# Twenty-two dummy products on TensorE ahead of the first expert tile

## The reference

```python
def _moe_ref(x, w_gate, w_local, w1, w2):
    ...
            h = np.maximum(x[b, s] @ w1[e], 0.0)
            out[b, s] = p[e] * (h @ w2[e])

def _moe2_ref(x, g_ln, w_ch1, w_ch2):
    ...
    xn = (x - mu) / np.sqrt(var + 1e-06) * g_ln
    ch = np.maximum(xn @ w_ch1, 0.0) @ w_ch2
    return (x + ch).astype(np.float32)
```

## Time and profile before

| | |
|---|---|
| median of three runs | 433.4 us |
| span of the profiled execution, first to last instruction | 428.4 us |
| rest of the time, by that median | 5.0 us |
| TensorE products, busy | 392.5 us (92%) |
| VectorE, ScalarE, GpSimd busy | 233.5, 139.4, 127.5 us |
| mean granted TensorE clock | 0.944 |

### The profile page before, as it was taken

The page is one execution under the profiler, slowest core; times in us unless marked ns, Lnnn a source line. Parts: engine busy times, 40 slices in busy tenths (PEclk is TensorE's granted clock), DMA queues, the critical chain, the costliest instruction groups (busy, mean ns, idle before and its releaser), DMA issues.

```text
span 428.4 us, 7294 instructions
## 1 busy us (share of the span) xinstructions
PE 392.5 (92%) x2640; PEld 372.0 (87%) x2640; DVE 233.5 (54%) x440; ACT 139.4 (33%) x283; POOL 127.5 (30%) x128
## 2 busy tenths in 40 slices
PE   6799999995049999999999999899999999999993
PEld 5799999894049999999999999788998899988993
DVE  6887879974406573663745769586303652133110
ACT  0424536320007254372553735452002220022000
POOL 4685653613705235053250521300100001100010
PEclk9999999955559999999999999999999999999998
DMA  7998984063534869577584270410010001000000
GB/s 114 154 248 209 249 213 73 20 227 124 203 116 148 256 228 364 178 271 261 201 314 159 102 261 1 128 59 2 18 38 18 0 2 37 27 13 2 18 20 37
DMA packets 62250, 54.77 MB, mean 128 GB/s; under 512 B 41216, under 2 KB 56960, under 8 KB 62208
## 3 DMA queue, kind: packets, MB, share of 16 engines
q1 hardware_dynamic: 47744, 19.58, 18.8%
q10 hardware_dynamic: 12032, 26.74, 18.1%
q0 software_dynamic: 2432, 7.92, 4.8%
HBM read 43.13 MB, written 11.10 MB: 127 GB/s over the span
## 4 chain that ended last, share of the span: by engine, by line
PE 82%; DVE 6%; issue 4%; DMA 3%; ACT 2%; SPq 1%; POOL 0%; DVEq 0%; ACTq 0%; POOLq 0%
PE bank L1200 21%; PE bank L1202 21%; PE bank L1201 21%; PE bank L1162 4%; PE bank L1159 3%; PE bank L1147 3%; PE bank L1137 2%; PE bank L1171 2%; PE bank L1113 2%; PE bank L1195 1%; DMA kn<-in_k 1%; PE bank L1126 1%; DVE split L365 1%; PE bank L1212 1%; DMA xrow<-xsort 1%
## 5 line engine op out<-in xcount | busy, mean ns | idle before, releaser
L360 ACT CAST split<-raw 128x1024 fp32r<-128x1024 f32 (+1 forms) x60 | 59.2, 1004 | 0.0
L1200 PE MATMUL bank<-xT,split 128*128 128x256 f32 x192 | 55.1, 287 | 2.1 <-DVE xT L901 2.1
L1202 PE MATMUL bank<-xT,split 128*128 128x256 f32 x192 | 54.8, 286 | 0.0
L1201 PE MATMUL bank<-xT,split 128*128 128x256 f32 x192 | 54.8, 286 | 0.0
L365 DVE TENSOR_TENSOR split<-raw,split 128x1024 fp32r<-128x1024 f32 (+1 forms) x40 | 52.9, 1337 | 1.8 <-ACT split L360 1.7
L590 POOL DMA_INDIRECT out<-orow,cpos x12 | 11.6, 970 | 133.4 <-DVE orow L1030 133.4
L1200 PE MATMUL bank<-split,h2T 128*128 128x384 f32 x144 | 48.7, 338 | 0.0
L1202 PE MATMUL bank<-split,h2T 128*128 128x384 f32 x144 | 48.2, 335 | 0.0
L1201 PE MATMUL bank<-split,h2T 128*128 128x384 f32 x144 | 48.1, 334 | 0.0
L365 POOL TENSOR_TENSOR split<-raw,split 128x1024 fp32r<-128x1024 f32 (+1 forms) x20 | 45.8, 2305 | 5.7 <-ACT split L360 3.4
L1042 DVE SCALAR_TENSOR_TENSOR h2T<-bank,h2T 128x512 fp32r<-128x512 f32 x36 | 24.9, 691 | 38.0 <-ACT h2T L702 37.8
(11 more groups left out here) (166 smaller groups left out, 764.3 us busy)
## 6 DMA issues: line engine op xcount, KB each, us to landing
raw<-in_w ACTq DMA_DIRECT2D x14, 1536.0 KB, 7.3
raw<-in_w_ch ACTq DMA_DIRECT2D x2, 2304.0 KB, 9.0
xsort<-zeros SPq DMA_DIRECT2D x8, 388.0 KB
X<-xsort SPq DMA_DIRECT2D x8, 388.0 KB, 5.8
ysort<-yrow POOLq DMA_DIRECT2D x8, 388.0 KB, 7.0
raw<-in_w SPq DMA_DIRECT2D x2, 1536.0 KB, 8.2
X<-ysort SPq DMA_DIRECT2D x3, 776.0 KB, 6.2
rn<-in_r SPq DMA_DIRECT2D x12, 192.0 KB, 4.8
```

Source lines behind the costliest of these rows:

```text
L360: act.copy(hi, src).then_inc(s_hi, 1)
L1200: pe.matmul(dst, stationary[0], moving[0], start=first, stop=False)
L1201: pe.matmul(dst, stationary[0], moving[1], start=False, stop=False)
L1202: return pe.matmul(dst, stationary[1], moving[0], start=False, stop=last)
```

## The change

A loop of 22 bf16 products is put on TensorE between `expert_regs` and the first tile's transposes. Each has `blank` (128x128 zeros) as its stationary operand and the same tile, repeated four times, as its 512 moving columns, and writes bank 0. Nobody reads what they write: the transposes overwrite it. They carry no wait and no signal.

```diff
     WARM_UP = 56
+    KEEP_WARM = 22
...
             pe.sem_inc(m_o, WT)
             tiles, before, _, behind, more = expert_regs(pe)
 
+            for _ in range(KEEP_WARM):
+                pe.matmul(bank[0][:], blank[:], blank[:].unsqueeze(1).broadcast_to([P, 4, P]), start=True, stop=True)
+
             def moe_transpose():
```

## The result

Ten executions of each gave a median of 435.86 us for the changed kernel and 433.5 us for the one before. The ratio of the two is 1.0067, with a 95% interval from 1.0048 to 1.0086: slower by 2.9 us, and clear of no change. One of the changed kernel's ten took 678.23 us at a mean granted clock of 0.548, and the ratio is of the other nine. Timed again in a later series, the changed kernel came to 436.43 us, ratio 1.0090 [1.0058, 1.0122].

What follows compares the result with a forecast made beforehand. TensorE was taken to set the end, busy 295.4 of 296.6 us from 125.22. Transposes 5.8 us later less 2.0 given back make +3.8, 428.4 to 432.2; with 5.0 around the span, 437.2 us, range 435.8 to 439.3.

Steps and rivals of the forecast that it cites:

- the forecast's own +3.0 to +5.0: The main case's range of loss in us at the end of the profiled execution, given 72 in 100.
- Where the dummies start: TensorE's hole before the first transposes: dummies start near 120.5 behind the tenth read; only 1.1 us to 121.59 is free.
- What they take: The 22 dummies: 9.6 products in 4.07 us, 12.4 in 2.80, 6.87 us in all; transposes 5.8 us later.
- What is given back: First transposes and expert products at full clock: 0.72 us plus 1.28 us, together 2.0 us.
- The rule of the Trainium skill: First six transposes: full clock does not engage, so the 0.72 us would be missing and the sum +4.5 us.
- The products' 1.28 us: First expert products: 13.7 take 1.64 us at full clock in place of 2.92, 1.28 us less.
- The clock that falls again: Rival, between dummies and first products: clock falls, +5.1, at worst +6.4 us, 438.5 to 439.8 us; 12 in 100.
- Absorbed downstream: Rival: TensorE's one later wait, on VectorE's normalised rows, absorbs up to 1.2 us, giving 436.0 us; 6 in 100.
- The sum: End of the profiled execution: 5.8 - 2.0 = +3.8 us, 428.4 to 432.2, giving 437.2 us.
- the 5.0 us between span and median: Time taken to lie around the profiled span by the median, added to the span to forecast the measured time.
- Faster, same: Rivals: dummies start at 113.3, hidden, 431.4 us, 3 in 100; start between 115.7 and 117.7, no change, 3 in 100.
- the estimate from the Trainium skill: The ten reads: about 200 ns per register load, ending at 115.3, dummies near 122.2; -1.4 us, 432.0 us.

Runs made afterwards that it cites:

- the run with narrow dummies: 22 dummies of 128 columns in place of 512, at the changed kernel's place behind the reads; 431.73 against 432.49 us, ratio 0.9981.
- The run with the start at 115.0: The changed kernel's 22 dummies behind the second of the ten reads in place of the tenth; 432.28 against 432.49 us, ratio 0.9993.

## Why the prediction was right, point by point

The mechanism was right: the dummies start behind the tenth read, run past the rows and are paid for on TensorE. Of the number, part is luck. The measured 435.86 us is 2.5 us above the 433.4 that the forecast started from; it lies 0.06 us above the lower end of the range, and below the forecast's own +3.0 to +5.0. That lower end is lower than its working gives: +3.2 less the half microsecond is +2.7, or 436.1 us, and the text has 435.8. The forecast of 437.2 us itself is 1.3 us too high.

**Where the dummies start.** Forecast: right behind the tenth read, near 120.5, with 1.1 us free. Measured: 120.5 in the later series, 122.5 in the first profile, whose attention ended 1.58 us later. Right, and the run with the 22 behind the second read shows that this start decides.

**What they take.** Forecast 6.87 us, with the rise after 4.07. Measured 6.76 and, in the later series, 7.41 us (the rise after 3.7 and 5.1), and 12.18 for 44 where the same rates give 6.87 + 22 x 0.226 = 11.8. The transposes came 5.95 and 6.55 us later against the last routing product; the forecast was 5.8.

**What is given back.** Forecast 2.0 us. Measured 2.0 where the clock stayed, 0.5 where it fell (299.91 less 297.92 and 299.41). Transposes 0.82 for 1.54 us, as forecast. The rule of the Trainium skill ("TensorE: Matmul & The Clock Gate", Part 4: PE-mode transpose) that the full clock does not engage for them is not borne out in any of the runs that reached them at 1.00. The products' 1.28 us: from the first product to the last of all, 295.0 us with the clock at 1.00 throughout against 296.28 before, 1.26 less.

**The clock that falls again.** A rival with 12 in 100, and the chance that I mis-sized. Four profiles reached the transposes at 1.00 with the pause behind them empty (the changed kernel twice, the one with 44 behind the reads, the 22 behind the second read), and the clock fell in three: in the pause in the last, 0.4 to 1.1 us behind the first product in the other two. I had argued from the earlier trace rows, a stretch with a pause of 1.7 us in which the clock stayed at 1.00. That was one execution. In five of the experiments' profiles the clock fell in this same stretch, between 11.0 and 11.6 us, and in the changed kernel's first at 13.6. The run with 22 ahead of the reads, for one:

```profile
7.70:12.10 4.40, 1.80 (x12) 0.94 1.26 193
```

The price was over-estimated in turn: a fall takes back 1.5 us (296.51 against 295.02), hardly more than the products' 1.3, and not up to twice that. With that pause filled the clock fell in neither of two profiles.

**Absorbed downstream.** This rival's 436.0 us is the number nearest to the measured one, but it is not what happened. The wait that was to absorb a part is as long as before in the changed kernel:

```profile
PE bank L1204 <- DVE split L934: 1.2, 1, 1.2
```

And in the later series' profile the stretch from the first expert product to the end differs from the kernel before's by the clock's share alone, 1.3 us.

**The sum.** Forecast +3.8 us; behind the last routing product the two profiles show +5.4 (with the fall) and +4.6 (without it), the medians +2.4 to +3.8, and by the ratio +2.9. What was weak is that every price was read from one execution. I took the 5.0 us between span and median for time around the span. The changed kernel's profiled execution took 437.12 us for a span of 435.5, 1.6 more. If the kernel before has the same around it, its profiled execution took 430.0 us, 3.4 below its median, and none of its 86 executions timed here was as short (the shortest took 430.37). The other profiles say which kind of execution that is: of these thirteen, the six whose clock fell early in the attention lie 0.1 to 2.9 us above their kernel's median, the seven without that fall 1.0 to 3.1 us below it. The kernel before's profile has no such fall. The two that are alike, it and the changed kernel's of the later series, are 434.24 less 430.0 = 4.2 us apart, and the medians of that series 3.8, the forecast's own number. Why the first series' medians stand only 2.4 apart is not shown. One thing that would make a loss smaller than in these profiles is a later request of the rows: 11.9 us behind the last routing product in the kernel before's profile, 11.9 to 13.1 in the others. In the run with narrow dummies the first products ran 5.6 us at 0.50 in place of 2.9, which leaves more for an early rise to give back. Both are arguments; the profiles of single executions can't settle them.

**Faster, same.** The prediction put the break-even at a start near 116.7. The run with the start at 115.0 lies on the winning side of it, and made no difference. By the sum it should have won 1.7 us; in its profile the clock fell, which is 1.5 of it. The reads took 7.2 to 7.6 us wherever the dummies stood behind them, 0.31 of each 0.7 being the load itself, so the estimate from the Trainium skill ("Runtime: NRT & Kernel Launch", section Instruction fetch mechanics), which would have had the kernel faster, falls.

## What to carry to other kernels

Work that is to fill a wait fills it only if it is issued when the wait begins: look at what the sequencer does in the hole, not at the array's idle time, for register reads hold back every instruction behind them. Filler goes between the reads, and it may last no longer than what it covers; what is longer is paid to the last microsecond on an engine that bounds the kernel. And keeping the clock up to the first real product takes filling every pause up to it: behind one empty pause of 2 us the clock fell in three of four profiles, and with it went most of what the filler had won. Where the clock can't be kept up all the way, 5 products in that one pause gave 1.4 us by the medians, with nothing else added. And prices read from one profile are prices of one kind of execution: compare its time with the median before adding them up.

## What the runs showed of the hardware

- TensorE's sequencer took 6.9 to 7.6 us for ten reads of a register with no products between them, 0.7 us each, of which the load itself is 0.31 (median).
- It goes on into register reads while the array still works on its queue, but only a limited way: behind 22 products the first read was not late, behind 44 it came at 116.8 with the counts ready at 114.8, behind 56 at 119.2 with the counts ready at 115.0.
- Behind the start of the same dummies, with TensorE idle for 8 to 14 us before, the clock rose after 2.8, 3.0, 3.7, 5.1 and 5.1 us in five profiles.
- The clock held through most of a pause of 3.4 us and fell 3.1 us into it, at 123.7, in the run with 44 ahead; in the run with 22 behind the second read it fell at 124.9, in the pause of 2.1 us. It fell once in the early attention in some executions and not in others of like kernels, which moves the last routing product from some 106.5 to 108.3 us.
